# Scores in two whole banks and a shared rest, and values, transposes and scores of a step moved together

## Chip, cores, metric

The kernel runs on one NeuronCore of one Trainium2 chip. The metric is the device time of one execution in microseconds, lower is better.

## What is computed

Top-k attention over four batches of eight heads, followed by two feed-forward layers over all 2304 tokens, everything in float32:

```python
B, H, S, D = 4, 8, 576, 64                       # q, k, v: [B, H, S, D]
scores = scale * np.matmul(q, k.transpose(0, 1, 3, 2))
kth = np.partition(scores, -32, axis=-1)[..., -32:-31]
scores = np.where(scores >= kth, scores, -1e9)
attn = softmax(scores)                            # max subtracted, 1e-9 added to the sum
x = np.matmul(attn, v)                            # -> [2304, 512]
h = x @ w_in;  g = np.maximum(0.01 * h, h);  y = g @ w_out        # layer 0, 512 -> 2048 -> 512
h = y @ w_in2; g = np.where(h >= 1, h, np.where(h <= -1, 0, (h + 1) ** 2 / 4)); out = g @ w_out2
```

## The kernel before

**Items and tiles.** Two heads make a pair (PAIRS = 4 in a batch). A head's 576 query rows are four blocks of 128 (MAIN = 512) and a rest of 64 (REST). An *item* is one block of rows of a pair: its scores are two tiles of 128 x 576, one for each head. The item of the rest rows is *mixed*: the 64 rest rows of both heads lie over each other in one tile. There are 80 items with 144 tiles. The items of a pair come in two groups (gp): blocks 0 and 1, then blocks 2, 3 and the mixed one; at the end of each group the product with V (`values`) is made. Item n has its tiles `first` to `last`.

**What happens to an item.** PE computes scores (`score`), ACT copies them to SBUF (`copy_scores`), DVE finds the 32 largest of each row with four MAX8 and three MATCH_REPLACE8 for each tile (lines 1022 and 1025) and marks what falls out (`find_drop`, L1031), POOL adds scores and marks (`mask`, L598), ACT takes the exponential (`exponential`, L873), DVE sums up and inverts the row sum (L1038, L1043), ACT scales the rows (`normalise`, L881), PE transposes them in 128 x 128 blocks (`transpose`, L713 to L720), ACT copies these to `p_t` and `p_rem` (`copy_transposed`, L889 to L896), PE multiplies with V (`values`, L736), ACT copies the result to x (`copy_values`, L910 and L912), and POOL makes its low part (`low_x`, L603).

**Feed-forward.** A float32 product is made as three products of a high and a low part (lines 777, 778, 785; high weight with high x, low weight with high x, high weight with low x, which is x minus its high part, made by POOL). The tokens go in seven chunks of 256, 320 or 384 columns. For each chunk, layer and block of 8 hidden slices there are 8 hidden units (12 products each, here written H) and 4 output units (24 products each, here written O). H01.3 is hidden unit 3 of layer 0, block 1. ACT reads a hidden unit's bank twice (L932/L933, or L936/L937), in layer 1 DVE (L1049), POOL (L619) and ACT (L946) finish it, and POOL makes the low part (L613). The first output unit of a block needs all eight hidden units before it; the first hidden unit of layer 1 needs layer 0's sums (DVE L1057, ACT L954, POOL L623). Units rotate through three PSUM banks `ps_f`.

**Steps.** All engines walk through the same 153 steps, in an order written out by hand for each engine. At step s, DVE is some two tiles ahead, POOL masks tile s-4, ACT takes the exponential of tile s-5, and an item is transposed at `out_step`, 6 or 7 steps after its last tile. `make_plan` gives each step the feed-forward units for which it has credit, in three groups `first`, `second`, `third` (mostly one unit each, and third often empty); where a unit needs the one before it, `first` ends ahead of it. READY[c] is the step from which chunk c can be fed; READY[0] is 22. Before it the steps have no units (the quiet steps), step 152 holds the units that are left. At step 21 the first three units (EARLY_UNITS) are begun with the three pairs that are there, and the fourth pair follows at step 22.

**Order on PE in a step with units, before.** In a step in which an item is transposed: scores, first, values, second, transposition, third. In others: first, scores, values, second, third. On ACT: copy of scores (in a step with a transposition), exponential, first, (scores), normalise the item of the next step, second, copy of values, copy of transposed, third.

**PSUM before.** Eight banks: `ps_s` two, `ps_t` two, `ps_av` one, `ps_f` three. The scores of an item are made in two halves of 288 columns each: the first in `ps_s`, the second in `ps_f` (the 11 items before feed-forward starts) or in `ps_t` (later, as `ps_late`). So the later items' scores share `ps_t` with the transposes: `score` waits for `p_t_copied`, and `transpose` for `scores_copied`. Of the bank `ps_av`, 320 columns hold the values and 128 (`ps_rem`) the last block of a transposition.

**DMA.** Weights are split into high and low at the start ("pieces", `high_piece` on ACT, `low_piece` on POOL L584, stored by SP) and streamed by SP from then on. The q and k of a pair lie in `kq` (1152 columns).

## Time and profile before

| | |
|---|---|
| time, median of 3 runs | 1212.53 us (1211.87 to 1213.77) |
| the profiled execution, its own time | 1213.45 us |
| span of the profiled execution | 1211.5 us |
| busy, share of span | PE 1116.4 us (92%), DVE 928.6 (77%), ACT 702.9 (58%), POOL 608.1 (50%) |
| chain that ended last | PE 69%, DVE 20%, POOL 4%, ACT 3%, issue 3% |

The page gives busy times for each engine: PE matmuls, PEld weight loads, DVE, ACT, POOL, SP. Matmuls are pipelined and their ends are modelled, so the time from one matmul's start to the next one's start says what a matmul costs in a row of them, and its listed duration is longer than that. The same holds in part for ACT and DVE instructions that follow each other. In a timeline a bracket behind a line holds the idle time of the engine before it and the instruction that ended it. A float32 matmul that is not of the feed-forward kind stands in the trace as two instructions.

### The profile page before, as it was taken

To read this page: it belongs to the slowest core of one execution; us is meant where nothing else is said; L and a number is where in the kernel's file an instruction comes from. 1 tells how busy PE (TensorE), PEld (TensorE's weight loads), DVE (VectorE), ACT (ScalarE), POOL (GpSimd) and SP (SyncE) were. 2 spreads that over 40 slices of the span, in tenths; PEclk is the share of its full clock that TensorE was granted. 3 is DMA by queue.
4 is the path that set the end of the run, shared out by engine and by line. 5 is a ranking of instruction groups with operands and counts; after the bars stand their busy time and mean duration, and the time that the engine had idled before them with its cause. 6 is when DMAs were issued, how large, how long until landed. Compare 5 with 4: busy or idle time off the path is not lost.

```text
span 1211.5 us, 21061 instructions
## 1 busy us (share of the span) xinstructions
PE 1116.4 (92%) x7360; PEld 1005.3 (83%) x7360; DVE 928.6 (77%) x2088; ACT 702.9 (58%) x1579; POOL 608.1 (50%) x582
## 2 busy tenths in 40 slices
PE   3546998979999999999999989999899999999998
PEld 2334987869989888888987878898789999999998
DVE  7999999979889999899989988969989005300244
ACT  5665877646667765666666755666765524312232
POOL 5674878735456644555545654445745323222322
PEclk9877999989999999999999999999999999999999
DMA  6887997856675688777676747445446677787774
GB/s 229 277 302 270 379 335 288 276 195 213 209 250 208 237 290 277 252 244 246 229 233 217 244 163 236 174 159 189 146 174 214 195 243 263 257 271 257 246 241 149
DMA packets 86792, 287.12 MB, mean 237 GB/s; under 512 B 9632, under 2 KB 13472, under 8 KB 86688
## 3 DMA queue, kind: packets, MB, share of 16 engines
q1 hardware_dynamic: 79200, 270.04, 64.5%
q10 hardware_dynamic: 7488, 15.73, 3.8%
q8 instruction: 60, 0.98, 0.3%
q14 instruction: 44, 0.36, 0.1%
HBM read 247.46 MB, written 38.27 MB: 236 GB/s over the span
## 4 chain that ended last, share of the span: by engine, by line
PE 69%; DVE 20%; POOL 4%; issue 3%; ACT 3%; DMA 1%; ACTq 0%; POOLq 0%; SPq 0%
PE ps_f L777 18%; PE ps_f L785 18%; PE ps_f L778 17%; DVE top L1022 7%; DVE work L1025 7%; PE ps_av L736 6%; DVE part_r L1049 3%; PE ps_s L692 2%; PE ps_t L713 2%; PE ps_t L692 2%; DVE drop L1031 2%; PE ps_t L719 2%; POOL gate L613 1%; POOL part_o L619 1%; POOL drop L598 1%
## 5 line engine op out<-in xcount | busy, mean ns | idle before, releaser
L1022 DVE MAX8 top<-work 128x8 f32<-128x576 f32 x432 | 309.3, 742 | 0.1
L785 PE MATMUL ps_f<-gate,w_ring 128*128 128x384 f32 (+2 forms) x896 | 283.4, 316 | 17.0 <-POOL gate L613 17.0
L777 PE MATMUL ps_f<-xy,w_ring 128*128 128x384 f32 (+2 forms) x896 | 289.2, 323 | 2.9 <-ACT xy L954 2.5
L598 POOL TENSOR_TENSOR drop<-scores,drop 128x576 f32<-128x576 f32 x144 | 207.9, 1444 | 166.8 <-DVE drop L1031 166.8
L777 PE MATMUL ps_f<-gate,w_ring 128*128 128x384 f32 (+2 forms) x896 | 287.8, 321 | 3.2 <-ACT part_o L933 1.9
L785 PE MATMUL ps_f<-xy,w_ring 128*128 128x384 f32 (+2 forms) x896 | 281.4, 314 | 6.2 <-POOL xy L603 4.4
L778 PE MATMUL ps_f<-gate,w_ring 128*128 128x384 f32 (+2 forms) x896 | 281.2, 314 | 0.0
L778 PE MATMUL ps_f<-xy,w_ring 128*128 128x384 f32 (+2 forms) x896 | 280.5, 313 | 0.0
L1025 DVE MATCH_REPLACE8 work<-top,work 128x576 f32<-128x576 f32 x288 | 212.7, 738 | 0.0
L785 PEld LDWEIGHTS ps_f<-gate,w_ring 128*128 128x128 f32 x896 | 170.6, 190 | 21.2 <-POOL gate L613 20.9
L777 PEld LDWEIGHTS ps_f<-xy,w_ring 128*128 128x128 f32 x896 | 169.9, 190 | 20.1 <-issue 11.5
L613 POOL TENSOR_TENSOR gate<-part_r,gate 128x384 fp32r<-128x384 f32 (+2 forms) x112 | 101.8, 911 | 168.8 <-ACT gate L937 168.6
L777 PEld LDWEIGHTS ps_f<-gate,w_ring 128*128 128x128 f32 x896 | 170.6, 190 | 16.7 <-issue 10.1
L1057 DVE TENSOR_TENSOR y_acc<-ps_f,y_acc 128x384 f32<-128x384 f32 (+2 forms) x56 | 27.7, 494 | 197.0 <-PE ps_f L785 196.9
L785 PEld LDWEIGHTS ps_f<-xy,w_ring 128*128 128x128 f32 x896 | 170.0, 190 | 7.9 <-POOL xy L603 4.6
L778 PEld LDWEIGHTS ps_f<-gate,w_ring 128*128 128x128 f32 x896 | 170.8, 191 | 0.0
L778 PEld LDWEIGHTS ps_f<-xy,w_ring 128*128 128x128 f32 x896 | 170.1, 190 | 0.0
L613 POOL TENSOR_TENSOR gate<-part_o,gate 128x384 fp32r<-128x384 f32 (+2 forms) x112 | 101.7, 909 | 81.1 <-ACT gate L946 81.0
L1049 DVE SCALAR_TENSOR_TENSOR part_r<-part_r 128x384 f32<-128x384 f32 (+2 forms) x112 | 74.9, 669 | 64.8 <-ACT part_o L933 64.8
L873 ACT ACTIVATE probs<-drop,neg_max 128x576 f32<-128x576 f32 x144 | 112.3, 780 | 19.7 <-issue 12.1
L881 ACT ACTIVATE probs<-probs,row_inv 128x576 f32<-128x576 f32 x144 | 104.8, 775 | 29.2 <-DVE row_inv L1043 29.1
L1022 DVE MAX8 top<-scores 128x8 f32<-128x576 f32 x144 | 107.0, 743 | 6.8 <-ACT scores L853 6.8
(91 smaller groups left out, 1833.0 us busy)
## 6 DMA issues: line engine op xcount, KB each, us to landing
w_ring<-w_split SPq DMA_DIRECT2D x412, 512.0 KB, 4.1
w_split<-w_ring SPq DMA_DIRECT2D x36, 512.0 KB, 6.9
raw<-wd SPq DMA_DIRECT2D x64, 256.0 KB, 5.1
w_split<-xy SPq DMA_DIRECT2D x28, 512.0 KB, 3.9
kq<-kqd ACTq DMA_DIRECT2D x12, 576.0 KB, 7.2
v_sb<-vd ACTq DMA_DIRECT2D x12, 320.0 KB, 4.0
out_t<-y_acc ACTq DMA_DIRECT2D x12, 192.0 KB, 4.0
kq<-kqd SPq DMA_DIRECT2D x3, 576.0 KB, 7.2
```

Source lines behind the costliest of these rows:

```text
L598: pool.tensor_tensor(slot, scores[:, it.n % S_SLOTS, t - it.first, :], slot, ALU.add).then_inc(masked, 1)
L613: pool.tensor_tensor(gate[:, 1, u.slot, cols], src[:, u.h % G_SLOTS, 0:u.width], gate[:, 0, u.slot, cols].bitcast(F32), ALU.subtract).then ...
L692: pe.matmul(out[:, 0, 0:PART], q[0:D, rows], k[0:D, c0:c1], start=True, stop=True)
L736: mm = pe.matmul(ps_av[a * D:(a + 1) * D, 0:width], w, x, start=c == 0, stop=c == KC)
L777: pe.matmul(out, w[:, 0, m], high, start=first, stop=False)
L778: pe.matmul(out, w[:, 1, m], high, start=False, stop=False)
L785: mm = pe.matmul(out, w[:, 0, m], low, start=False, stop=end)
L873: act.activation(probs[:, it.n % P_SLOTS, a * S:(a + 1) * S], drop[:, t % D_SLOTS, :], ACT.Exp, bias=neg_max[:, t % 8:t % 8 + 1], scale=SCALE,
L881: op = act.activation(p, p, ACT.Copy, scale=row_inv[:, it.n % T_SLOTS, a:a + 1])
L1022: dve.max(top[:, t % T_SLOTS, 8 * r:8 * r + 8], source(t, r)).then_inc(dve_step, 1)
L1025: dve.match_replace(work[:, t % 2, :], top[:, t % T_SLOTS, 8 * r:8 * r + 8], source(t, r), LOWEST).then_inc(dve_step, 1)
L1049: dve.scalar_tensor_tensor(out=r, in0=r, scalar=1.0, in1=r, op0=ALU.min, op1=ALU.mult).then_inc(curved, 1)
```

## The change

Scores of an item now use the two banks of `ps_s` whole: one matmul of 512 columns for each head. The 64 last columns of both heads are made by a third matmul of 128 columns over all 128 partitions into `ps_rem`, against a block-diagonal copy of k's rest with zeros, which the host adds to `kq` (now 1216 columns). The transposes have `ps_t` for themselves. `ps_rem` is shared by the rest of the scores and the last block of the transposes, and its bank also by the values; so a rest waits for `rem_copied` and `x_copied`, the last block of a transposition for `x_copied` and `scores_copied`, and `values` for all of them. ACT copies a two-tile item's scores in one copy of 2 x 512 columns and one of 128; `work` is now behind the slots of `scores` so that this copy's view fits. `copy_transposed` copies the rest first.

In steps with units, PE now runs: first, values, transposition, scores, second, third. ACT: exponential, first, copy of values, copy of transposed, copy of scores, second, normalise the next step's item, third. Scores of later items are moved to the latest step with a transposition at or before their first tile. The values of a group, from the fifth on, are made in the step in which the next item is transposed (one step later than before), which moves READY to 22, 45, 61, 81, 117, 133, 152 (before 22, 44, 60, 80, 116, 132, 152) and so shifts the units among the steps. Item 10 is scored at step 22 (before at 18).

In the quiet steps: the first early unit is begun ahead of the transposition of step 21, the second ahead of the last values; ACT takes the exponential before it copies transposes, and copies values a step later; the last four held pieces are made at steps 19 and 21 (before 21 and 22); POOL's `low_x` of the fourth pair stands at step 20, ahead of the masks of steps 20 and 21 and of the pieces of step 21 (before at 22, behind them).

```diff
-PART = S // 2
+KQ = S + MAIN + 2 * REST
...
 def values_step(gp):
+
     last = ITEM_OF[LAST_OF_GROUP[gp]]
-    return out_step(last) + (not starts_early(gp))
+    if starts_early(gp):
+        return out_step(last)
+    return out_step(ITEMS[last.n + 1]) if last.n + 1 < len(ITEMS) else out_step(last) + 1
...
 def score_step(it):
-    if it.first < READY[0] - 1:
+
+
+    if it.n < FIRST_LATE:
         return max(0, it.first - 2, ITEMS[it.n - S_SLOTS].last + EXP_LAG if it.n >= S_SLOTS else 0)
-    return max(it.first - it.mixed, READY[0])
+    with_others = [s for s in OUT_AT if READY[0] <= s <= it.first]
+    return max(with_others[-1:] + [READY[0] + it.n - FIRST_LATE])
...
             for s, (first, second, third) in enumerate(PLAN):
-                if s == READY[0]:
+                if s == READY[0] - 2:
                     low_x(CHUNKS[0].last_gp)
+                if s == READY[0] - 1:
+                    for i in lowered_pieces(s):
+                        low_piece(i)
                 if s < READY[0] and s >= MASK_LAG:
                     mask(s - MASK_LAG)
...
                 need(pe, scores_copied, 2 * it.n)
...
+                else:
+                    pe.matmul(ps_s[:, 0, :], q[0:D, rows], k[0:D, :], start=True, stop=True)
+                    pe.matmul(ps_s[:, 1, :], q[D:P, rows], k[D:P, :], start=True, stop=True).then_inc(scores_done, 1)
+                need(pe, rem_copied, issued["transposes"])
+                need(pe, x_copied, issued["values"])
+                if it.mixed:
+                    pe.matmul(ps_rem[D:P, :], q[:, rows], rest, start=True, stop=True)
+                    pe.matmul(ps_rem[0:D, :], q[:, rows], rest, start=True, stop=True).then_inc(scores_done, 1)
+                else:
+                    pe.matmul(ps_rem, q[:, rows], rest, start=True, stop=True).then_inc(scores_done, 1)
+                issued["scores"] += 1
...
+                need(pe, x_copied, issued["values"])
+                need(pe, scores_copied, 2 * issued["scores"])
+                if it.mixed:
                     pe.transpose(ps_rem[0:REST, :], p[:, MAIN:S], ident[:, :]).then_inc(transposed, 1)
...
                 for u in first:
                     feed(u)
-                if not scores_first(s):
-                    for it in SCORED_AT[s]:
-                        score(it)
-                if s in VALUES_AT and s >= READY[0]:
+                if s in VALUES_AT:
                     values(VALUES_AT[s])
-                for u in second:
-                    feed(u)
-                if s - 1 in VALUES_AT and s < READY[0]:
-                    values(VALUES_AT[s - 1])
                 if s in OUT_AT:
                     transpose(OUT_AT[s])
-                if s == READY[0] - 1:
-                    begin(EARLY_UNITS[0])
-                    values(VALUES_AT[s])
-                    for u in EARLY_UNITS[1:]:
-                        begin(u)
-                for u in third:
+                for it in SCORED_AT[s]:
+                    score(it)
+                for u in second + third:
                     feed(u)
...
+                else:
+                    both = scores[:, slot:slot + 2 * (MAIN + P)].rearrange("p (a n) -> p a n", a=2)
+                    act.activation(both[:, :, 0:MAIN], ps_s[:, :, :], ACT.Copy).then_inc(scores_copied, 1)
+                    act.wait_ge(scores_done, 2 * it.n + 2)
+                    act.activation(scores[:, slot + MAIN:slot + MAIN + P], ps_rem, ACT.Copy).then_inc(scores_copied, 1)
...
+                if done:
+                    copy_transposed(done)
+                for it in SCORED_AT[s]:
+                    copy_scores(it)
                 for u in second:
                     event(u)
-                if s in VALUES_AT and s >= READY[0]:
-                    copy_values(VALUES_AT[s])
-                if done and s >= READY[0]:
-                    copy_transposed(done)
+                if s + 1 in OUT_AT:
+                    normalise(OUT_AT[s + 1])
                 for u in third:
                     event(u)
```

## Rows read from the trace of the kernel before

**Rows 1.** The page, part 2: busy tenths of PE and DVE in 40 slices.

```profile
PE   3546998979999999999999989999899999999998
...
DVE  7999999979889999899989988969989005300244
```

**Rows 2.** Windows: stretch, length, busy us of each engine (instructions), granted clock, DMA.

```profile
116.20:121.00 4.80, 4.73 (x18) 3.47 (x19) 4.80 (x10) 3.33 (x9) 4.80 (x6) 0.51 0.97 329
```

**Rows 3.** Waits of PE from 112 us on: total us, times, longest; largest and fourth row.

```profile
PE ps_f L785 <- POOL gate L613: 17.0, 15, 2.6
PE ps_s L692 <- ACT p_rem L890: 5.3, 4, 1.4
...
PE ps_f L777 <- ACT xy L954: 2.5, 2, 2.2
```

**Rows 4.** Timeline of PE around the start of feed-forward: start, duration, instruction, [idle before].

```profile
116.27 0.58 PE L785 MATMUL ps_f<-xy,w_ring 128*128 128x256 f32 x1 [4.44 <-POOL xy L603]
116.78 0.84 PE L692 MATMUL ps_s<-kq 64*128 64x288 f32 x1
...
130.55 0.60 PE L713 MATMUL ps_t<-ident,probs 128*128 128x128 f32 x4
```

**Rows 5.** Chain of waits, 80 to 125 us: start, duration, what.

```profile
113.07 2.46 POOL xy L584 x2
115.53 0.69 POOL xy L603
```

**Rows 6.** Timelines of DVE and ACT, 98 to 124 us.

```profile
98.63 1.02 ACT L889 ACTIVATE p_t<-ps_t 128x1024 f32<-128x1024 f32 x1 [0.54 <-PE ps_av L720]
...
100.61 0.17 DVE L1038 TENSOR_SCALAR row_eps<-row_sum 128x2 f32<-128x2 f32 x1 [2.49 <-ACT probs L873]
...
109.93 0.37 ACT L912 ACTIVATE x_raw<-ps_av 128x256 f32<-128x256 f32 x1
...
123.81 0.15 DVE L1043 RECIPROCAL row_inv<-row_eps 128x2 f32<-128x2 f32 x1
```

**Rows 7.** Timeline of PE around one item's scores, 412 to 415 us.

```profile
412.69 0.28 PE L778 MATMUL ps_f<-xy,w_ring 128*128 128x256 f32 x1
412.81 0.28 PE L785 MATMUL ps_f<-xy,w_ring 128*128 128x256 f32 x1
413.01 0.51 PE L692 MATMUL ps_s<-kq 64*128 64x288 f32 x1
...
413.36 0.40 PE L692 MATMUL ps_s<-kq 64*128 64x288 f32 x1
...
413.60 0.40 PE L692 MATMUL ps_t<-kq 64*128 64x288 f32 x1
...
414.19 0.42 PE L777 MATMUL ps_f<-gate,w_ring 128*128 128x320 f32 x1
```

**Rows 8.** Timeline of PE in the quiet steps: scores right behind a transposition.

```profile
89.80 0.42 PE L720 MATMUL ps_av<-ident,probs 128*128 128x128 f32 x1
90.15 0.74 PE L698 MATMUL ps_s<-kq 64*64 64x288 f32 x1
```

**Rows 9.** Timeline of PE: transposition of one item, 335 to 337 us.

```profile
335.98 0.60 PE L713 MATMUL ps_t<-ident,probs 128*128 128x128 f32 x4
...
336.88 0.39 PE L777 MATMUL ps_f<-gate,w_ring 128*128 128x320 f32 x1
```

**Rows 10.** Timeline of ACT in fed steps: reading units, normalising, copies of values.

```profile
276.50 0.44 ACT L936 ACTIVATE part_r<-ps_f 128x320 f32<-128x320 f32 x1
276.82 0.45 ACT L937 ACTIVATE gate<-ps_f 128x320 fp32r<-128x320 f32 x1
277.13 1.47 ACT L881 ACTIVATE probs<-probs,row_inv 128x576 f32<-128x576 f32 x2
278.47 0.45 ACT L936 ACTIVATE part_r<-ps_f 128x320 f32<-128x320 f32 x1
...
268.81 0.44 ACT L910 ACTIVATE xy<-ps_av 128x320 fp32r<-128x320 f32 x1 [1.84 <-PE ps_av L736]
```

More of the change, by code:

```diff
@@ L678, in _ @@
         def _(pe):
+            issued = {"scores": 0, "transposes": 0, "values": 0}
             def score(it):
@@ L1017, in source @@
             def source(t, r):
[L1018 to L1019 removed]
+                return work[:, t % 2, :] if r else tile_scores(t)
             def top8(t, r):
```

197 lines of the change are left out of this document (93 added, 104 removed).

## The prediction

> **What bounds the kernel now.** I read the busy tenths first, then the waits of PE, then the timelines where those waits lie. PE is 92% of the span busy (the table), and its row of tenths shows 3 to 6 in the first three slices and almost only 9 behind the fifth [rows 1]. So there are two parts. The first 116 us are the quiet steps: DVE is at 9 there and sets the pace, PE idles. From then on it is PE: the waits of PE from 112 us on are eleven rows, together 36.4 us of 1100, with 17.0 us for low parts from POOL as the largest and 5.3 us for copies of transposes as the second [rows 3]. A PE that hardly waits can win only what the waits hold, and loses at once whatever is added to its own row. DVE is at 8 and 9 up to the thirty-first slice [rows 1], so it is a near second: a PE that runs ahead of DVE gets its time back as a wait.
>
> **The start.** In the quiet steps two things are mended. (a) The low part of the fourth pair is queued on POOL behind a mask and two pieces: pieces from 113.07 for 2.46, then 0.69 for `low_x` [rows 5], though its input was ready at 110.30 (109.93 and 0.37) [rows 6]; PE waits 4.44 us for it [rows 4]. Ahead of the masks it ends at about 110.3 + 0.7 = 111.0, which is 5.2 us earlier. What is queued behind it are the masks of steps 20 and 21 and with them two exponentials; DVE needs those only two tiles later, so nobody waits. (b) ACT's exponential of the first chunk's last tile stands behind a copy of transposes that waits for PE (98.63) [rows 6]; DVE waits 2.49 us for its sum. With the exponential ahead, and the mixed item's scores (at 90.15 [rows 8]) and their four copies on ACT moved out to step 22, that wait goes. DVE, the norm, the transposition of step 21, the values and x come 2.5 us earlier. (c) One early unit's nine products, 1.1 us at the full clock and 1.9 at the half, are done while PE waits for that transposition. Together PE's stalled product at 116.27 [rows 4] can run at about 108.0, that is 8.3 us earlier.
>
> But DVE is only 2.5 us earlier, and it is next. Item 8 is transposed in step 24. Its inverse came at 123.81 + 0.15 [rows 6], now 121.5; two normalising copies, 1.47 us [rows 10], give 123.0. Before, PE came to this transposition at 130.55 [rows 4], behind two units of the step; now it stands behind the first alone. PE gets there at 108.0 + 1.4 (scores of item 10) + 0.8 (rest of the early units) + 4 units of 12 x 0.12 = 1.44 + 1.3 (item 11) = 117.3 and waits 5.7 us. What it had done before at 130.55 and lacks now are two scores and a unit, 1.3 + 1.3 + 1.44 = 4.0, so it is level at 127.0, 3.5 us ahead. The clock takes a part back: behind the wait of 4.44 us the granted clock was 0.51, the lower of the two levels (1.2 of 2.4 GHz), for the 4.8 us up to 121.0 [rows 2], some 2.3 us lost. I expect one such wait instead of one such wait, perhaps a longer one. I take 2.5 us won. Bounds: 0 (DVE gains nothing) and 9.2 (8.3 + 2.3 - 1.4, if the wait for item 8 is not there).
>
> **Waits on `ps_t` that go.** Scores no longer wait for the copy of transposes: 5.3 us in four waits [rows 3], and by the smaller rows of the same view 0.8 and 0.2 us (once a transposition, once mixed). 6.3 us are won. One or two of them lie in a stretch at the half clock; 1 us more for that. Bounds 4 and 9.
>
> **The scores' own time.** From the last product's start at 412.81 to the next one's at 414.19 are 1.38 us; less the product's own 0.12 (412.69 to 412.81, 256 columns) an item costs 1.26 us [rows 7]. In it four instruction pairs of 288 columns take 0.24 each (413.36 to 413.60), 0.96; the two heads run side by side. 288 columns in 0.24 us are 0.83 ns a column, so now 2 x 512 columns take 0.85 and the rest's 2 x 128 take 0.21, 1.07: 0.11 more for each item. 69 items are scored in the fed part before, 70 now: +7.5 us. Then the borders. Into the scores PE loses 413.01 - 412.81 - 0.12 = 0.08 and 0.35 - 0.24 = 0.11 [rows 7]. At the half clock the first of these took 116.78 - 116.27 less a product's 0.21, 0.30 [rows 4]; behind a transposition 90.15 - 89.80 less a block's 0.20, 0.15 [rows 8]. So scores right behind a transposition save half of the entry, 0.08 at the full clock. 67 items are so placed, 5.4 us; against it, 19 pairs of neighbouring values and scores before shared a border of 0.1, and 16 mixed items now switch once more, by 1 us; the transposition itself costs 336.88 - 335.98 = 0.90 [rows 9] in either place, and the exit to the rest and to the products is the same 0.1. I take 3 us back: +4.5. Bounds -2 and +11.
>
> The Trainium skill, "TensorEngine Tiling (Array Packing)", section Key Properties, says that changing the tiling mode, not just the tile, drains the engine. The trace agrees in kind: a transposition (128x128, like the products) has no border cost, scores (64x128) and values (128x64) have. By that rule the one stretch saves no switch, since the transposition in its middle is in the products' mode and the rest of the scores is too; I count 172 switches in the fed steps before and about 209 after, at 0.1 us each +3.7 us in place of the -3.
>
> **PE now comes to its transposition early, ACT late.** This is the new wait. Before, ACT normalised between first and second of the step before, and PE transposed behind second of the step. Now ACT normalises behind second, and PE transposes behind first. Between them lie, on PE, one unit (and the values, where there are any); on ACT the two reads of second's unit, 277.13 - 276.50 = 0.63, and the normalising, 278.47 - 277.13 = 1.34 of occupancy plus its tail [rows 10], some 2.3 us with the hand-over. A hidden unit of 256 columns takes 1.44 us [rows 7]; with the width, one of 320 about 1.8 and one of 384 about 2.1; an output unit twice that. So PE waits 0.2 to 0.65 us where both units are hidden ones, third is empty and no values stand between, and nothing elsewhere. By the new steps these are items 21, 25, 35, 38, 61, 65, 69, 75 and 78: 4.5 us with what layer 1 adds (one more ACT copy). Queued behind the waiting transposition on PE are the scores and all units of the step. Bounds 1 and 30 (0.7 at each of the 42 transpositions without values).
>
> **The shared bank.** In the 27 stretches with values the last block of the transposition waits for both copies of the values. ACT starts on them 0.05 us behind the end of the values and needs some 0.8 for both (268.81, 0.44 long) [rows 10], and PE has only eight blocks of 0.1 us in between: 0.1 us each, 2.7 us. The rest of the scores waits for the copy of the last block; ACT is free 0.8 to 1 us behind first and PE has 0.85 us of main scores, so this is mostly covered; where layer 1 makes ACT wait for POOL it is not: 1 us. Sum 3.5, bounds 0 and 12.
>
> **Covers that move.** Scores and transposes also covered the waits for gates and for layer 0's sums. In the new order the first hidden unit of layer 1 loses its cover in chunks 0, 1, 2 and 4, and the output units of chunk 1's second block lose theirs; an uncovered one costs up to the 2.2 us that chunk 3's did [rows 3]. Chunk 3 and the output units of chunk 0 gain one. Net +1, bounds -5 and +5. Host and DMA: `kq` is 5.5% longer, the first load ahead of the first score too, 0.1 to 0.2 us, in the start's rounding. ACT's copies of scores hold as many columns as before in as many instructions; nothing moves. Each step's stream of weights on SP follows its units; its loads are eight pieces ahead.
>
> **Sum.** -2.5 - 6.3 - 1.0 + 4.5 + 4.5 + 3.5 + 1.0 = +3.7 us on the profiled execution's 1213.45 (span 1211.5 and 1.95 around it), which is 0.9 above the median: 1216 against 1212.53.
>
> **Rivals.** (1) Faster: ACT keeps up. In the trace it often idles ahead of a copy of transposes, so the two terms of ACT (8.0) may be 2, and if item 8's wait costs less by 2 to 3 us the sum is -5 to -8: 1206. Against it: ACT's normalising has a fixed place now, behind a read it can't do earlier. It decides from 0.2 us a stretch. (2) The switches are paid in full, as the page has it: +6.7 on the forecast, 1222. For it: T to S is shown at the half clock alone. (3) Slower: PE waits at most transpositions without values, since ACT's reads stand behind POOL and DVE in layer 1: 42 x 0.7 = 29 in place of 4.5 would give 1240; half of that, 1230. Against it: the table of steps has nine such places. (4) The change does nothing that counts: the waits that it removes return as waits for gates, as PE comes earlier to the same DVE and POOL: 1212.5 within 2.
>
> **Chances.** Forecast 0.43, (1) 0.33, (2) 0.08, (3) 0.08, (4) 0.08. Range 1203 to 1228: all of (1) and (2), a part of (3), the bounds of the terms partly cancelling. What a measurement of this kernel can tell from no change is about 0.2%, 2.4 us. Faster: (1) and the low end of the forecast, 0.36; same: (4) and a quarter of the forecast, 0.21; slower 0.43.
>
> **What would show it.** Right: `low_x` gone from the waits and a wait of 4 to 6 us for item 8's probabilities near 118 to 123 us with a half clock behind it; no wait of L692 for p_rem; main scores 0.43 us apart; waits of the transposition for ACT's probs in fed steps, 4 to 6 us in all, and of the last block for x_raw. Wrong: PE's fed stretch shorter by more than 5 us; PE waiting for DVE throughout; more than 10 us of waits for probs.

## The result and the profile after

| | before | after |
|---|---|---|
| median (range of the runs) | 1212.2 us (1211.5 to 1213.8) | 1245.8 us (1242.6 to 1248.4) |
| ratio to before, 95% interval | | 1.0276 [1.0256, 1.0296] |
| the profiled execution, its span | 1213.45, 1211.5 | 1248.37, 1246.5 |
| PE busy, share of span | 1116.4 (92%) | 1142.4 (92%) |
| DVE, ACT, POOL busy | 928.6, 702.9, 608.1 | 927.0, 707.0, 607.6 |

The change costs 33.6 us. The forecast was +3.7, with an upper end of +15.5. It had the sign, but neither the time nor the range. The four executions of the kernel after fall in two pairs, 1242.6 and 1243.4 us (mean granted clock 0.977 and 0.974) and 1248.2 and 1248.4 (0.962 in both); the profile is of the second pair, and what sets the pairs apart wasn't found. Lines of the new kernel are shifted by up to 5 in PE's part: products are L780, L781 and L788, the main scores L694 and L695 (mixed items L691 and L692), the rest of the scores L702 (mixed L699 and L700), the transposition L710 and L715 with its last block L721, values L741. On ACT the copy of the last block is L895 (L899 for an item of one tile), that of the values L916 and L918.

The tenths of PE and DVE in 40 slices (each now 31.2 us long):

```profile
PE   4547998989999999999999989998999999999998
DVE  7999989989789888899968977977889204320144
```

The picture is that of [rows 1]: PE at 9, DVE a near second with somewhat less in each slice. Nothing has become idle; the kernel does more on PE for the same result. The waits of PE from 104 us to the end, with total us, how often, and the longest:

```profile
PE ps_f L788 <- POOL gate L610: 15.2, 11, 2.5
PE ps_av L702 <- ACT p_rem L895: 8.2, 6, 3.1
PE ps_t L710 <- ACT probs L887: 6.8, 12, 1.7
PE ps_s L694 <- ACT scores L859: 4.8, 4, 1.6
PE ps_av L721 <- ACT x_raw L918: 3.9, 3, 3.1
PE ps_f L780 <- ACT xy L960: 3.6, 2, 2.3
PE ps_av L702 <- ACT p_rem L899: 2.9, 2, 2.4
```

Against [rows 3] the 5.3 us of scores for `p_rem` at the head of a step are gone, as forecast, and the 17.0 for gates are 15.2. New are four things: the rest of the scores waits for the copy of the last block, 8.2 + 2.9; the transposition waits for its probabilities, 6.8; the main scores wait for the copy of the mixed item that was scored just before, 4.8; the last block waits for the copy of the values, 3.9. These five rows make 26.6 us.

Waits alone don't make the loss. One stretch with values, a transposition and scores, on PE's timeline (start, duration, instruction):

```profile
229.32 0.28 PE L788 MATMUL ps_f<-gate,w_ring 128*128 128x256 f32 x1
229.53 2.37 PE L741 MATMUL ps_av<-p_t,v_sb 128*64 128x320 f32 x16
...
232.37 0.66 PE L710 MATMUL ps_t<-ident,probs 128*128 128x128 f32 x4
...
233.30 0.33 PE L721 MATMUL ps_av<-ident,probs 128*128 128x128 f32 x1
233.56 0.69 PE L694 MATMUL ps_s<-kq 64*128 64x512 f32 x1
...
234.09 0.59 PE L694 MATMUL ps_s<-kq 64*128 64x512 f32 x1
...
234.62 0.49 PE L702 MATMUL ps_av<-kq 128*128 128x128 f32 x2
234.86 0.36 PE L780 MATMUL ps_f<-xy,w_ring 128*128 128x256 f32 x1
```

From the last product's start to the next one's are 234.86 - 229.32 = 5.54, less the product's 0.12: 5.42, without any wait. I took this figure, the excess of a stretch over its products, for all stretches of each kernel. Medians of stretches without a wait, in us (S scores of one item, T transposition, V values; 320 columns for V):

| stretch | before | sum of before's parts | after |
|---|---|---|---|
| S alone | 1.26 | | none |
| T alone | 0.90 | | 0.90 |
| V alone | 2.93 | | 2.93 |
| T then S | | 0.90 + 1.26 = 2.16 | 2.38 |
| V, T, S | 4.10 (S and V without T) | 4.10 + 0.90 = 5.00 | 5.43 |

From 112 us on, all such stretches together take 237.4 us before and 279.4 after. The 42 us more are 20 of own time (40 stretches T, S at 0.22 and 27 with values at 0.42), 19.6 of waits (26.9 after, 7.3 before), 1.4 for item 10's scores, which now lie in this part, and about 1 at the half clock.

This figure leaves out what a stretch does to the product behind it. Behind values, and behind scores of the old form, the first product takes 0.10 us more than its columns; behind a transposition, and behind the rest of the scores, 0.08. Before, behind the transposition of [rows 9], the first product of 320 columns takes 0.23 and the next one 0.14:

```profile
336.88 0.39 PE L777 MATMUL ps_f<-gate,w_ring 128*128 128x320 f32 x1
337.11 0.30 PE L778 MATMUL ps_f<-gate,w_ring 128*128 128x320 f32 x1
337.25 0.31 PE L785 MATMUL ps_f<-gate,w_ring 128*128 128x320 f32 x1
```

Joined stretches have fewer such products, 75 in place of 146, and that gives 6.9 us back (13.8 to 6.9). So the own time grows by about 13 us, not by 20. With the product behind: T and S apart cost 0.98 + 1.36 = 2.34 before, and T then S costs 2.46 now; S with V, and T apart, cost 4.20 + 0.98 = 5.18, and V, T, S costs 5.51.

Over the whole span of 35.0 us more, the first product of feed-forward runs 6.6 us earlier (97.7 against 104.3). The waits of PE from there on grow from 36.4 us to 53.5, of which 2.7 belong to item 7's transposition, which stood ahead of the first product before. The stretches without their waits, but with the product behind, grow from 246.7 to 265.1. The other products that take over 1.6 times the time of their columns grow from 82 to 142, and what they lose from 10.8 us to 16.7. -6.6 + 17.1 + 18.4 + 5.9 = 34.8. The last term is the clock behind long waits. Four stretches of such products, 5.5 us in all, have hardly a counterpart before. They stand behind the waits for the rest's bank at 423.69 (1.65 us long), 673.23 (2.38) and 702.98 (1.97), and for the values' copy at 538.66 (3.07); the windows behind these (columns as in [rows 2]) have granted clocks of 0.52 to 0.65:

```profile
423.70:427.00 3.30, 3.30 (x17) 3.30 (x18) 3.30 (x10) 2.58 (x6) 3.30 (x4) 0.57 0.02 7
539.00:543.00 4.00, 4.00 (x19) 3.24 (x20) 4.00 (x9) 2.63 (x5) 3.64 (x5) 0.65 0.00 0
673.40:677.00 3.60, 3.60 (x15) 3.60 (x16) 0.62 (x1) 1.70 (x4) 2.00 (x2) 0.54 0.00 1
703.90:707.00 3.10, 3.10 (x15) 3.10 (x14) 3.10 (x8) 1.38 (x3) 3.10 (x3) 0.52 0.02 5
```

Followed along the run by the same number of products, after stands to before as: 168 products, -0.7 us; 504, +11.3; 672, +4.5; 1176, +10.4; 2184, +20.5; 3192, +28.3; 4032 and all later ones, +35.0. The order of units differs between the two, so that single points jump, but the loss grows over the whole fed part while items remain, and stops with them.

### The profile page after: what moved, and what is told of

Read it like the earlier page. It is cut to its first block, busy times and chain, and to the rows that moved or that the text cites. A ratio compares the mean times of both kernels' runs of the same rounds, so it can differ in the third digit from the quotient of the medians.

```text
span 1246.5 us, 20807 instructions
## 1 busy us (share of the span) xinstructions
PE 1142.4 (92%) x7200; PEld 992.6 (80%) x7200; DVE 927.0 (74%) x2088; ACT 707.0 (57%) x1578; POOL 607.6 (49%) x582
## 4 chain that ended last, share of the span: by engine, by line
PE 68%; DVE 18%; POOL 6%; ACT 4%; issue 3%; DMA 1%; ACTq 0%; POOLq 0%; SPq 0%
PE ps_f L788 17%; PE ps_f L780 17%; PE ps_f L781 17%; DVE top L1028 7%; DVE scores L1031 6%; PE ps_av L741 5%; PE ps_s L694 4%; PE ps_t L710 3%; DVE part_r L1054 2%; POOL gate L610 2%; PE ps_av L702 2%; DVE drop L1036 2%; PE ps_t L715 2%; POOL drop L595 1%; POOL part_o L616 1%
## 5 line engine op out<-in xcount | busy, mean ns | idle before, releaser
L1028 DVE MAX8 top<-scores 128x8 f32<-128x576 f32 x576 | 405.2, 743 | 7.6 <-ACT scores L863 7.5
L1031 DVE MATCH_REPLACE8 scores<-top,scores 128x576 f32<-128x576 f32 x432 | 317.7, 739 | 0.0
L788 PE MATMUL ps_f<-gate,w_ring 128*128 128x384 f32 (+2 forms) x896 | 283.6, 317 | 15.2 <-POOL gate L610 15.2
L780 PE MATMUL ps_f<-xy,w_ring 128*128 128x384 f32 (+2 forms) x896 | 287.7, 321 | 6.4 <-ACT xy L960 3.6
L788 PE MATMUL ps_f<-xy,w_ring 128*128 128x384 f32 (+2 forms) x896 | 284.2, 317 | 2.4 <-POOL xy L620 2.3
L780 PE MATMUL ps_f<-gate,w_ring 128*128 128x384 f32 (+2 forms) x896 | 285.2, 318 | 0.0
L781 PE MATMUL ps_f<-xy,w_ring 128*128 128x384 f32 (+2 forms) x896 | 283.0, 316 | 0.0
L781 PE MATMUL ps_f<-gate,w_ring 128*128 128x384 f32 (+2 forms) x896 | 282.0, 315 | 0.0
L1062 DVE TENSOR_TENSOR y_acc<-ps_f,y_acc 128x384 f32<-128x384 f32 (+2 forms) x56 | 27.8, 496 | 217.3 <-PE ps_f L788 217.3
L788 PEld LDWEIGHTS ps_f<-gate,w_ring 128*128 128x128 f32 x896 | 171.2, 191 | 18.2 <-POOL gate L610 18.2
L780 PEld LDWEIGHTS ps_f<-xy,w_ring 128*128 128x128 f32 x896 | 172.3, 192 | 9.9 <-ACT xy L960 4.1
L788 PEld LDWEIGHTS ps_f<-xy,w_ring 128*128 128x128 f32 x896 | 172.5, 193 | 4.6 <-POOL xy L620 4.4
L781 PEld LDWEIGHTS ps_f<-xy,w_ring 128*128 128x128 f32 x896 | 172.4, 192 | 0.0
L780 PEld LDWEIGHTS ps_f<-gate,w_ring 128*128 128x128 f32 x896 | 171.6, 192 | 1.0 <-issue 0.7
L781 PEld LDWEIGHTS ps_f<-gate,w_ring 128*128 128x128 f32 x896 | 171.5, 191 | 0.0
L887 ACT ACTIVATE probs<-probs,row_inv 128x576 f32<-128x576 f32 x144 | 104.5, 772 | 24.7 <-DVE row_inv L1048 24.7
L879 ACT ACTIVATE probs<-drop,neg_max 128x576 f32<-128x576 f32 x144 | 111.3, 773 | 10.8 <-issue 5.0
L942 ACT ACTIVATE part_r<-ps_f 128x384 f32<-128x384 f32 (+2 forms) x112 | 49.8, 445 | 95.3 <-PE ps_f L788 93.2
```

Of the source, the lines that this page charges most:

```text
L780: pe.matmul(out, w[:, 0, m], high, start=first, stop=False)
L781: pe.matmul(out, w[:, 1, m], high, start=False, stop=False)
L788: mm = pe.matmul(out, w[:, 0, m], low, start=False, stop=end)
L879: act.activation(probs[:, it.n % P_SLOTS, a * S:(a + 1) * S], drop[:, t % D_SLOTS, :], ACT.Exp, bias=neg_max[:, t % 8:t % 8 + 1], scale=SCALE,
L887: op = act.activation(p, p, ACT.Copy, scale=row_inv[:, it.n % T_SLOTS, a:a + 1])
L1028: dve.max(top[:, t % T_SLOTS, 8 * r:8 * r + 8], source(t, r)).then_inc(dve_step, 1)
```

## The experiments

Times are medians. Each ratio is to the kernel before, measured beside it on the same chip. Experiments 1 to 4 ran on one chip (before 1212.6 us), 5, 6, 7 and 9 on another (before 1213.8), 8 on a third (before 1213.2). So a difference between two experiments of different chips is uncertain by 1 to 2 us; where it matters, the difference of the ratios is given too.

**1. The quiet steps alone.** The kernel before with only the changes to the steps ahead of feed-forward.

```diff
-                if s == READY[0]:
+                if s == READY[0] - 2:
                     low_x(CHUNKS[0].last_gp)
...
+                if s == READY[0] - 1:
+                    begin(EARLY_UNITS[0])
...
```

> The kernel before with the quiet steps of the change alone (low part of the fourth pair ahead of the masks, exponential ahead of the copy of transposes, first early unit ahead of the transposition, pieces at 19 and 21); scores, PSUM and fed steps as before. Theory A (the start gains what DVE gains, 2.5 us): 1209 to 1211. Rival B (the gain of the start is given back to DVE and POOL at once): 1212 within 1. Rival C (the start carries a part of the 33 us): 1216 or more. PE's wait of 4.4 us for L603 goes in all three.

Measured 1208.8 us, ratio 0.9972 [0.9962, 0.9982], 3.8 below before's 1212.6. So these changes help, and nothing of the loss is theirs; theory A (1209 to 1211) is met within 0.2. The product that stood at 116.27 [rows 4] now runs at 108.41, and no row of its waits names the fourth pair's low part (L603). Part of these 7.9 us is given back at once: at the next item's scores PE waits 3.7 us for ACT's copy of scores (L865), which it didn't before. The largest rows in the fed part are the old ones:

```profile
PE ps_f L789 <- POOL gate L613: 16.9, 16, 2.6
PE ps_s L696 <- ACT p_rem L895: 5.3, 4, 1.4
```

**2. No third matmul.** The kernel after without the rest matmul and its waits. What is left out: the last 64 columns of the scores aren't computed, other data stand in their place.

```diff
-                need(pe, rem_copied, issued["transposes"])
-                need(pe, x_copied, issued["values"])
...
-                    pe.matmul(ps_rem, q[:, rows], rest, start=True, stop=True).then_inc(scores_done, 1)
...
```

> The changed kernel without the third matmul of the scores (the last 64 columns of both heads are not computed; ACT copies other columns in their place) and without the waits in front of it. Theory D (the form of the scores is the cause: the rest's own time, a border more and its waits for the shared bank): each transposition with scores behind it falls from 2.4 us to about 2.05, 70 times 0.33 is 23 us, and the 11 us of waits of L702 go: 1210 to 1216. Rival E (the order is the cause, transpositions ahead of ACT and covers that moved): 1232 or more.

Measured 1231.8 us, ratio 1.0156 [1.014, 1.0172]: 14 below after, at rival E's end and outside theory D's 1210 to 1216. The matmul itself takes 0.24 us (234.62 to 234.86 above), but without it the stretches' own time falls by 12.5 us only (table below), not by 70 times that. Its two rows of waits are 11.1. So 23.6 us are taken away, the slow products lose 3.3 less, and 14 are won. The waits of this kernel, 12.0 us more in the other rows, say where the remainder went:

```profile
PE ps_f L780 <- POOL gate L610: 21.7, 16, 3.4
PE ps_t L702 <- ACT probs L876: 7.1, 12, 1.9
PE ps_s L694 <- ACT scores L850: 6.3, 4, 1.9
```

Gates rise from 15.2 to 21.7, the copy of scores from 4.8 to 6.3, x (3.6 to 4.8) and the values (3.9 to 4.7) by 2.0 together: about 10 of the 12. The shared rest is therefore no more than half of the loss, and a PE that comes earlier gives back part of what it wins.

**3. New form, old order.** The kernel after with the order of a step as before: scores at the head in steps with a transposition, values and transposition around second, ACT's order to match, and the old steps of scores and values.

```diff
-    if starts_early(gp):
-        return out_step(last)
-    return out_step(ITEMS[last.n + 1]) if last.n + 1 < len(ITEMS) else out_step(last) + 1
+    return out_step(last) + (not starts_early(gp))
...
-    with_others = [s for s in OUT_AT if READY[0] <= s <= it.first]
-    return max(with_others[-1:] + [READY[0] + it.n - FIRST_LATE])
+    return max(it.first - it.mixed, READY[0] + it.n - FIRST_LATE)
...
+                if s in OUT_AT:
+                    for it in SCORED_AT[s]:
+                        score(it)
                 for u in first:
                     feed(u)
...
+                for u in second:
+                    feed(u)
                 if s in OUT_AT:
                     transpose(OUT_AT[s])
-                for it in SCORED_AT[s]:
-                    score(it)
-                for u in second + third:
+                for u in third:
...
```

> The changed kernel with the old order of the fed steps: scores at the head of a step with a transposition, values and scores together in the others (values first), transposition behind second, normalising ahead of second, old steps of scores and values. Scores keep two banks and the shared rest. Theory D (form): each item of scores still has three matmuls and borders, 70 times 0.2 to 0.3: 1222 to 1232, hardly any waits of L702. Rival E (order): 1212 to 1218.

Measured 1218.6 us, ratio 1.0044 [1.0028, 1.006], between theory D (1222 to 1232) and rival E (1212 to 1218) and nearer to E. The form costs 9.8 us over experiment 1, and the order with its steps 27 more. Of the rows of after for `p_rem`, `probs` and the mixed item's copy 0.2 is left, and the values' copy has one of 0.7:

```profile
PE ps_av L699 <- ACT x_raw L921: 0.7, 1, 0.7
```

One item's scores in this kernel, to lay beside [rows 7]:

```profile
411.19 0.28 PE L785 MATMUL ps_f<-xy,w_ring 128*128 128x256 f32 x1
411.40 0.69 PE L691 MATMUL ps_s<-kq 64*128 64x512 f32 x1
...
411.94 0.59 PE L691 MATMUL ps_s<-kq 64*128 64x512 f32 x1
...
412.46 0.49 PE L699 MATMUL ps_av<-kq 128*128 128x128 f32 x2
412.70 0.39 PE L777 MATMUL ps_f<-gate,w_ring 128*128 128x320 f32 x1
412.93 0.30 PE L778 MATMUL ps_f<-gate,w_ring 128*128 128x320 f32 x1
```

412.70 - 411.19 - 0.12 = 1.39, where before took 1.26: 0.13 more for an item of two tiles. The product behind takes 0.08 more than its columns where before had 0.10, so the item costs 0.11 more in all. A mixed one takes 1.46, 0.20 more, and the same behind it. Some 55 of the one and 15 of the other are 9.1 us, against 9.8 measured. The two agree only roughly by cause: by the table below the stretches' own time grows by 12.4, part of it at the lower clock, and the waits fall by 3.5, since the 6.3 us for copies of transposes go and 3.1 us in which values and a transposition wait for `p_t` come.

**4 to 6. The order, part by part.** Three kernels: after with second between transposition and scores (the waits of the form stay, the neighbourhood goes); after with transposition and scores adjacent but behind second, ACT normalising ahead of second as before, and the old steps of values; and experiment 1 with the transposition ahead of second and the normalising behind it, in the old form.

```diff
                 if s in OUT_AT:
                     transpose(OUT_AT[s])
+                for u in second:
+                    feed(u)
                 for it in SCORED_AT[s]:
                     score(it)
-                for u in second + third:
+                for u in third:
...
```

> The changed kernel with the unit group second between the transposition and the scores. ACT then has a unit's time to copy the last block ahead of the rest of the scores. Theory F (the stretch itself makes the waits for the shared bank): waits of L702 for p_rem, 11 us, and for doubled scores go, and with them some half clock: 1230 to 1235; a border into scores from a product costs no more than one from a transposition (0.26 us start to start). Rival: the waits move to other places, 1243 or more.

Measured 1233.2 us, ratio 1.0174 [1.0158, 1.019], as theory F has it. Scores cost 1.39 again and the rest's waits for `p_rem` fall from 11.1 to 1.7, but the transposition is still early:

```profile
PE ps_t L710 <- ACT probs L889: 5.8, 11, 2.3
...
PE ps_s L694 <- ACT scores L861: 4.6, 3, 1.5
PE ps_av L721 <- ACT x_raw L920: 3.5, 2, 3.0
```

The second of the three, against after:

```diff
-    if starts_early(gp):
-        return out_step(last)
-    return out_step(ITEMS[last.n + 1]) if last.n + 1 < len(ITEMS) else out_step(last) + 1
+    return out_step(last) + (not starts_early(gp))
...
+                for u in second:
+                    feed(u)
                 if s in OUT_AT:
                     transpose(OUT_AT[s])
                 for it in SCORED_AT[s]:
                     score(it)
-                for u in second + third:
+                for u in third:
...
+                if s + 1 in OUT_AT:
+                    normalise(OUT_AT[s + 1])
+                for u in second:
+                    event(u)
...
```

> Scores in two banks and a shared rest, with scores right behind the transposition as in the changed kernel, but both behind second, and normalising ahead of second, as before (the steps of values as before too). It differs from the old order (1218.6) by the neighbourhood of transposition and scores, and from the changed kernel (1245.8) by the place of the transposition. Theory G (the two parts of the order add): 1229 to 1233, with waits of L702 for p_rem of some 10 us and none of L710 for probs. Rival H (the rest waits only because the transposition comes early): 1219 to 1224, hardly a wait for p_rem.

Measured 1229.5 us, ratio 1.0118 [1.0095, 1.0141], as theory G has it. The expectation leaves out one difference to experiment 3: this kernel has the new steps of scores. No wait for probabilities is left, and those for the last block's copy are all there:

```profile
PE ps_av L700 <- ACT p_rem L895: 8.7, 5, 3.1
...
PE ps_s L692 <- ACT scores L859: 4.6, 3, 1.6
PE ps_av L697 <- ACT p_rem L895: 2.5, 2, 2.1
```

The third, against experiment 1:

```diff
-                for u in second:
-                    feed(u)
+                if s >= READY[0]:
+                    if s in OUT_AT:
+                        transpose(OUT_AT[s])
+                    for u in second + third:
+                        feed(u)
+                    continue
...
```

> The kernel before with the quiet steps of the change (1208.8) and old scores in halves, but in fed steps the transposition stands ahead of second and normalising behind second, as in the change. It has no shared rest. Theory I (a transposition that comes early waits for ACT, with 5 to 8 us of waits for probs and some half clock behind them): 1215 to 1219. Rival J (the early transposition does harm only through the shared bank): 1208 to 1211.

Measured 1213.5 us, ratio 0.9994 [0.9985, 1.0004]: 4.7 over experiment 1 by the medians, 2.7 by the ratios, between theory I (1215 to 1219) and rival J (1208 to 1211). This isn't the price of a late ACT alone. Of the transpositions' 16.6 us of waits only 2.6 name probabilities:

```profile
PE ps_t L717 <- issue: 14.0, 14, 4.8
...
PE ps_t L717 <- ACT probs L890: 2.6, 5, 0.9
```

In all 14 cases of the first row the transposition starts 0.09 to 0.10 us behind the end of ACT's last copy of an item's scores (the longest at 208.05, behind the copy L869 that ends at 207.95). In the old form the two share `ps_t`, and a transposition that comes early meets this. On the other side the waits for gates fall from 16.9 to 12.1 and those for `p_rem` from 5.3 to 1.4. So the 4.7 is a balance of other causes, and the new form, where the transposes have `ps_t` for themselves, hasn't got the largest of them.

All kernels in the same terms, in us, from the profiled executions. "Own" is the stretches without waits, with the product behind them, what they lose at the lower clock included; "slow" is what the other products of over 1.6 times their columns' time lose:

| kernel | span | first product at | waits from there on | own | slow |
|---|---|---|---|---|---|
| before | 1211.5 | 104.3 | 36.4 | 246.7 | 10.8 |
| experiment 1 | 1208.7 | 96.7 | 38.6 | 248.6 | 11.5 |
| 6, early transposition, old form | 1211.2 | 97.6 | 39.8 | 250.7 | 9.8 |
| 3, new form, old order | 1218.5 | 96.9 | 35.1 | 261.0 | 12.0 |
| 5, adjacent, behind second | 1228.5 | 98.6 | 40.4 | 261.9 | 14.0 |
| 4, second between | 1230.7 | 98.1 | 44.5 | 264.7 | 9.8 |
| 2, no third matmul | 1231.5 | 97.5 | 54.4 | 252.6 | 13.4 |
| 7, one item at a time | 1236.9 | 97.7 | 46.6 | 265.2 | 13.8 |
| after | 1246.5 | 97.7 | 53.5 | 265.1 | 16.7 |

From experiment 3 to after the order costs 28.0: 18.4 of waits, 4.7 of slow products, 4.1 of own time, 0.8 at the start. It is a price of waits, and hardly one of neighbours.

By the medians, transposition and scores adjacent cost +10.9 over experiment 3 (experiment 5; by the ratios 9.0), and the early transposition with the late normalising +14.5 (experiment 4). Both added to 1218.6 give 1244.0, and after has 1245.8. That this comes out so closely is in part luck. Both kernels have the new steps of scores too, so both have the doubled scorings of experiment 7 (4.6 us of waits in each), which the sum counts twice and after has once; and experiment 4 has the new steps of values besides. Taken once, the parts fall short of after by some 6 us, which they cost only together. Three rows of experiment 4 that experiment 3 lacks, or has at 0.7, are 3.5 for the values' copy, 4.6 for the mixed item's copy and 1.7 for `p_rem`.

**7. One item at a time.** In after three steps score two items one behind the other, a mixed one first. On after's timeline, PE and ACT:

```profile
348.88 1.02 ACT L896 ACTIVATE p_t<-ps_t 128x1024 f32<-128x1024 f32 x1
...
349.78 0.59 ACT L855 ACTIVATE scores<-ps_s 64x512 f32<-64x512 f32 x1
...
351.23 0.22 ACT L859 ACTIVATE scores<-ps_av 64x64 f32<-64x64 f32 x1
...
351.59 0.66 PE L694 MATMUL ps_s<-kq 64*128 64x512 f32 x1 [1.55 <-ACT scores L859]
```

The second item needs the whole of `ps_s`, which the first one holds until ACT has made its 1.02 for `p_t` and four copies. This kernel puts the second item into the step of its first tile.

```diff
-    return max(with_others[-1:] + [READY[0] + it.n - FIRST_LATE])
+    step = max(with_others[-1:] + [READY[0] + it.n - FIRST_LATE])
+    if it.n > FIRST_LATE and score_step(ITEMS[it.n - 1]) >= step:
+        return it.first
+    return step
```

> The changed kernel, but where two items would be scored in one step (56, 92, 128) the second is scored at its first tile's step. Expected: the wait of L694 for L859, 4.8 us in all, goes: 1239 to 1242. If its cover is needed elsewhere: 1244 or more.

Measured 1239.1 us, ratio 1.0202 [1.0184, 1.022], 6.7 below after (9.0 by the ratios), as expected. Of the row of 4.8 only 0.2 is left, and no other grew by more than 0.5. So the doubled scorings cost 6.7; of the 9.6 by the profiled spans 6.9 are waits and 2.9 slow products (table above).

**8. The rest first.** Experiment 3 with the rest matmul and its copy ahead of the two main ones, to see whether the border between the products' mode and the scores' is cheaper on one side than on the other.

> The kernel with two banks and a shared rest in the old order (1218.6, an item of scores 1.39 us), but in each item the rest, a 128x128 matmul like the products, is made ahead of the two main ones (64x128), so that a stretch of scores changes the array's mode twice as before, with the last change at its end. Theory K (a change of mode costs 0.1 us, wherever it stands): three borders stay two, an item costs 1.39 still or 0.05 less, 1215 to 1219. Rival L (what the rest costs beside its columns is the wait in front of its weight load): 1.27 an item, 1210 to 1213.

Measured 1247.4 us, ratio 1.0274 [1.0255, 1.0294]: both theories missed by 30 us, and in a part that neither spoke of. The scores' own time is 1.37 in place of 1.39, so the border has no cheap side. What changed is in the waits:

```profile
PE ps_av L693 <- ACT x_raw L921: 16.0, 16, 1.7
...
PE ps_av L690 <- ACT x_raw L921: 2.6, 3, 0.9
```

The rest shares its bank with the values. Where scores follow values, it now comes first and waits for both copies of the values, 19 times for 18.6 us; in experiment 3 the main scores covered all but 0.7 of this. In the quiet steps the same costs 7.8 us up to the first product, and the other 3 are small rows. So the main scores, 1.06 us long (411.40 to 412.46), are the cover under which the shared bank can work at all.

**9. A better kernel.** Experiment 1 keeps one row of [rows 3], the 5.3 us of scores for `p_rem`. It arises where the step before has a transposition and no third unit, so that scores at the head follow it directly. There the scores go behind first.

```diff
-    return s in OUT_AT
+    return s in OUT_AT and not (s - 1 in OUT_AT and s > READY[0] and not PLAN[s - 1][2])
```

> The kernel before with the quiet steps of the change (1208.8), and in steps 42, 78 and 114, where scores at the head stand right behind the last step's transposition, they are made behind first instead. The three waits of 1.4 us for p_rem, 4.1 us, and the half clock behind one of them should go: 1203.5 to 1205.5. Rival: PE then waits as long for gates: 1208 to 1209.

Measured 1204.1 us, ratio 0.9917 [0.9902, 0.9932]: 0.8% below before, as expected, and faster than both kernels. The row for `p_rem` has shrunk to 1.2. The wait that the change was to remove by a new use of the banks goes, for the larger part, with one unit put between.

## Why the prediction was right or wrong

**The start: right, but for the size of one wait.** -2.5 was forecast, experiment 1 measures -3.8 (-3.4 by the ratio). The stalled product was worked out at 108.0 and is at 108.41 there; item 8's transposition at 123.0, and it is at 123.42 in after, against 130.55 [rows 4]. The wait in front of it was forecast at 5.7 us. It is 1.72, since PE meets a gate first and waits 2.55 there:

```profile
119.47 0.39 PE L780 MATMUL ps_f<-xy,w_ring 128*128 128x256 f32 x1 [2.55 <-ACT gate L943]
...
123.42 1.12 PE L710 MATMUL ps_t<-ident,probs 128*128 128x128 f32 x4 [1.72 <-ACT probs L887]
```

The half clock behind waits came as in [rows 2]; the window from 119.4 to 127.6 (columns as there) has a granted clock of 0.58, and the next one, to 135.0, has 1.00:

```profile
119.40:127.60 8.20, 6.42 (x27) 4.45 (x27) 8.20 (x19) 7.10 (x18) 7.55 (x8) 0.58 1.02 401
```

**Waits on `ps_t` that go: right.** -6.3 forecast; the row of L692 is gone.

**The scores' own time: wrong, by some 9 us.** +4.5 was forecast, 13 to 14 came, and the bound of 11 was too low. The form was right: 0.11 an item was forecast, and 0.11 came, with 0.20 for a mixed one, 9.1 in all where the forecast had 7.5 and 1 for the mixed ones. The step that failed is "so scores right behind a transposition save half of the entry". It was read from two pairs of rows at different places, at the half clock behind a wait [rows 4] and in the quiet steps [rows 8], where the scores are those of a mixed item (64x64), another shape. At the full clock the timeline of after has the last block at 233.30 and the main scores at 233.56: 0.26, less a block's 0.10, is a border of 0.16, where the entry from products had 0.08 [rows 7] and has 0.09 in experiment 3. In exchange no product stands behind the transposition and loses its 0.08. So T and S of the new form cost 0.98 + 1.47 = 2.45 apart and 2.46 together: nothing is saved, and nothing is paid. The 67 places cost 1.2 us (0.01 each, 0.03 with values) in place of the 5.4 saved, 6.6 of the miss. The rest is the border that values and scores shared: V and S of the old form cost 3.03 + 1.36 = 4.39 apart and 4.20 together, so each of the 19 pairs saved 0.19 and not 0.1, and a transposition now stands between them, 3.6 us in place of 1.9. 9.1 + 1.2 + 3.6 = 13.9. A slip of 0.5 comes with it: the terms that the prediction names add up to 5.0, and it took 4.5. The choice to take 3 us back rested on rows of another state of the engine; the row at the full clock didn't exist in before, so the two ends (0.08 saved, nothing saved, something paid) should have been kept open and the nearest one at the full clock, no saving, taken. The sign "main scores 0.43 us apart" failed too: they are 0.53 apart (233.56 to 234.09), since the 0.11 behind the entry, which the prediction had itself read, falls there.

The Trainium skill, "TensorEngine Tiling (Array Packing)", section Key Properties, has a change of tiling mode drain the engine, which gave +3.7 for the borders. Rival 2 went by it. It was nearer than the forecast: all but the form came to +4.8, where the forecast had -3. It was right in that the neighbourhood saves nothing, but it counts borders as equal and has none between a transposition and products, both 128x128. The prediction says that the trace agrees, "a transposition has no border cost"; it looked at the entry alone, and the product behind a transposition takes 0.08 us more (336.88 to 337.11 above).

**Early transposition, late ACT: right in kind and size.** 4.5 us at nine places was forecast. The waits for probabilities are 6.8 in twelve: 1.7 at item 8, which the forecast has in the start; 3.4 at exactly the nine items that it names; and 1.65 at two that it doesn't, items 15 and 58. Experiment 6 does this part alone in the old form, but its +4.7 comes mostly from another wait and confirms nothing here. Rival 3, with 29 us or half of it by this mechanism, was wrong in the mechanism, though its upper time, 1240, is the nearest number in the prediction.

**The shared bank: wrong, 15.0 in place of 3.5.** The bound was 12. Two steps failed. The first is "ACT is free 0.8 to 1 us behind first and PE has 0.85 us of main scores, so this is mostly covered; where layer 1 makes ACT wait for POOL it is not: 1 us". The exception was seen and its price was not. Eight waits carry the 11.1 us, and four of them, 1.65 to 3.06 long, carry 9.1. In three of these four ACT stands behind reads of layer 1 that wait for POOL; in the fourth, at 673.23, it has waited 3.97 us for layer 0's sum from DVE (L1062). ACT and PE of after:

```profile
699.67 0.27 PE L721 MATMUL ps_av<-ident,probs 128*128 128x128 f32 x1
...
699.87 0.44 ACT L938 ACTIVATE part_r<-ps_f 128x320 f32<-128x320 f32 x1 [0.41 <-POOL gate L610]
...
700.52 0.78 ACT L879 ACTIVATE probs<-drop,neg_max 128x576 f32<-128x576 f32 x1
...
701.27 0.47 ACT L952 ACTIVATE gate<-part_o 128x320 fp32r<-128x320 f32 x1
701.99 0.44 ACT L938 ACTIVATE part_r<-ps_f 128x320 f32<-128x320 f32 x1 [0.24 <-POOL gate L610]
...
702.64 0.28 ACT L895 ACTIVATE p_rem<-ps_av 128x128 f32<-128x128 f32 x1
...
702.98 0.49 PE L702 MATMUL ps_av<-kq 128*128 128x128 f32 x2 [1.97 <-ACT p_rem L895]
```

When PE has made the last block, the reads of two units still stand before its copy on ACT, each pair held up by POOL's gate, with an exponential and a copy of a gate (L952) between them. Only then comes the copy of 0.28 us; PE waits 1.97 for it, and the whole step is queued behind. Before the change ACT was late as well, if at other items: by the timelines it starts this copy over 2 us behind the last block at 8 items before and at 6 after. Nobody needed it so soon then. The second step is the 0.1 us for each stretch with values: in 24 of the 27 nothing is seen, and three make 3.9, one of them 3.07 long by the same cause (ACT's copies of the values at 537.95 and 538.21, behind the same sequence). A mean over stretches was priced where a few late ones carry the cost.

**The doubled scorings: missing.** The prediction followed "scores are moved to the latest step with a transposition" for each item by itself, and didn't see that two items then fall into one step with one pair of banks. Experiment 7 prices this at 6.7 us.

**The clock behind the new waits: missing.** The prediction had the lower clock at the start, and 1 us of it that goes with the waits on `ps_t`; behind the waits that it foresaw for ACT it put nothing. The slow products lose 5.9 us more than before, and 5.5 us of such products stand behind four waits for the shared bank.

**Covers: right.** +1 forecast; the rows of waits within the products, without the stalled product's 4.4, are 24.7 before and 23.9 after, -0.8. What the bound hid is the feedback of experiment 2: with the rest and its waits gone the gates' row is 21.7, not 15.2.

**The rivals.** (1), 1206, fell with ACT's two terms, 21.8 in place of 8.0. (2), 1222, was near for the borders, and had nothing of the waits. (3) had a wait of PE for ACT as the main cost, with the wrong receiver: not the transposition for probabilities, but the shared bank. (4) fell. What was to show the prediction wrong, over 10 us of waits for probabilities, didn't occur; the waits came from a place for which I had named only the size.

The sum as measured, by medians from 1212.6: start -3.8, form +9.8, order with its steps +27.2, 1245.8. How the last splits is shown by its rows and by experiment 7 (6.7 of it), not by experiments 4 and 5 as a clean sum. By the rows the largest miss is the shared bank, 11.5 us; then the own time, some 9, the doubled scorings, and the clock.

## What to carry to other kernels

Two users of one bank make two engines keep step: price this wait by how late the releasing engine is in its worst layer, and see which work lies between (here the main scores, 1.06 us, hide a copy of 0.28, but not an ACT that is 2 to 3 us late). A wait of 1.65 to 3.07 us cost more than itself here: the granted clock in the windows behind it was 0.52 to 0.65. If PE is the bound, count its mode borders for each pair of neighbours at the full clock, with what the instruction behind loses, and take no saving that only rows at another clock show. Where a small wait is to be removed, try first to put one independent unit between the two; here that won 4.7 us (6.7 by the ratios), and a new layout of the banks cost 9.8, and 33.6 with the order that was to go with it.

## What the runs showed of the hardware

- Borders on PE at the granted clock of 1.00: products (128x128) to scores (64x128) 0.08 to 0.09 us, transposition to scores 0.16.
- The instruction behind a border pays too. The product behind values (128x64) or behind the old scores takes 0.10 us more than its columns, behind a transposition or the rest of the scores, 128x128 like itself, 0.08. So a transposition with products on both sides isn't free: it costs 0.90 and 0.08 behind it.
- Behind the first instruction of the scores there is a loss of 0.10 to 0.11 us, whatever its width: 0.35 for 288 columns where the next take 0.24 [rows 7]; 0.53 or 0.54 for 512, where 0.83 ns a column make 0.43. The last instruction of the main scores loses 0.09 to 0.10 against what follows in both forms (413.85 to 414.19 is 0.34 before, 411.94 to 412.46 is 0.52 in experiment 3). Both losses come once for a stretch, which is why fewer, wider instructions saved nothing.
- Behind single waits of PE of 1.65 to 3.07 us the granted clock was 0.52 to 0.65 over the next 3.1 to 4.0 us.
- Why a transposition makes the entry into scores 0.08 longer and the product behind it 0.08 slower was not separated: no run changed the transposition itself.
